# Splitting the second MoE layer's weights in another order, and waiting for the last scatters on another engine

## The reference

```
attn: scores = q k^T / 8;  keep scores >= max - tau;  softmax;  times v        4 x 8 heads, 576 x 64
moe : expert = argmax(xn @ en^T / tau);  out = gate * relu(x @ w1[e]) @ w2[e]   2304 tokens, 512 -> 1024 -> 512, 8 experts
last: h = x @ w_in;  g = h * tanh(log1p(exp(min(h, 20))));  out = g @ w_out      2304 tokens, 512 -> 2048 -> 512
```

## Time and profile before

| | |
|---|---|
| median of three runs | 1065.5 us |
| the profiled execution's own time | 1065.5 us |
| its span | 1063.9 us |
| PE busy | 1023.2 us (96%) |
| DVE / ACT / POOL busy | 625.7 / 505.5 / 587.7 us |
| mean granted TensorE clock | 0.987 of full |

### The profile page before, as it was taken

How to read it: one execution, slowest core, us unless ns; L and a number is a source line. 1 busy time by engine, 2 the same in 40 slices (tenths; PEclk the granted TensorE clock), 3 DMA queues, 4 the chain that set the end, 5 groups by cost and what they waited for, 6 DMA issues and landing times.

```text
span 1063.9 us, 20987 instructions
## 1 busy us (share of the span) xinstructions
PE 1023.2 (96%) x6712; PEld 850.1 (80%) x6712; DVE 625.7 (59%) x1484; ACT 505.5 (48%) x1020; POOL 587.7 (55%) x672
## 2 busy tenths in 40 slices
PE   7999999999966999899999999999999999999996
PEld 5777777777634888788888889999999999999995
DVE  6998989898764222122222226776676676666653
ACT  5777777777653222222222224555545545555442
POOL 3344444444345868677660627776556565565564
PEclk9999999999987999999999999999999999999999
DMA  8165425441065899998871736400000100000000
GB/s 200 40 169 161 120 81 152 127 125 44 12 220 149 247 287 279 293 295 266 291 240 47 264 104 208 119 31 21 27 14 31 31 10 20 30 30 0 9 22 31
DMA packets 97526, 128.87 MB, mean 121 GB/s; under 512 B 34400, under 2 KB 51808, under 8 KB 96928
## 3 DMA queue, kind: packets, MB, share of 16 engines
q1 hardware_dynamic: 72544, 66.54, 21.8%
q0 software_dynamic: 18880, 53.22, 15.8%
q10 hardware_dynamic: 6016, 7.96, 2.1%
HBM read 111.70 MB, written 16.00 MB: 120 GB/s over the span
## 4 chain that ended last, share of the span: by engine, by line
PE 59%; POOL 4%; DMA 4%; issue 2%; DVE 2%; ACT 1%; another core or an unknown queue 0%; POOLq 0%; SPq 0%; ACTq 0%; DVEq 0%
PE ps L1110 18%; PE ps L1111 18%; PE ps L1112 18%; DMA stage<-w 4%; POOL wl L594 3%; PE ps L1136 1%; PE ps L1048 1%; POOL wh L605 1%; PE ps L1185 1%; PE ps L1106 1%; POOL xs_far L631 1%; PE ps L1058 1%; ACT junk L824 1%; PE ps L997 0%
## 5 line engine op out<-in xcount | busy, mean ns | idle before, releaser
L594 POOL TENSOR_TENSOR wl<-stage,wh 128x512 fp32r<-128x512 f32 x128 | 162.8, 1294 | 56.0 <-DMA stage<-w 50.1
L708 POOL TENSOR_TENSOR mg<-mw,mr 128x384 f32<-128x384 f32 x96 | 117.3, 1222 | 73.7 <-DVE mr L1545 73.2
L766 ACT ACTIVATE ex<-sc,rmin 128x576 f32<-128x576 f32 x144 | 111.6, 776 | 78.0 <-DVE sc L1316 78.0
L714 POOL TENSOR_TENSOR gl<-mg,gh 128x384 fp32r<-128x384 f32 x96 | 98.6, 1028 | 79.1 <-ACT gh L902 78.2
L1110 PE MATMUL ps<-yth,winh 128*128 128x384 f32 x384 | 130.9, 341 | 0.0
L1112 PE MATMUL ps<-yth,winl 128*128 128x384 f32 x384 | 129.5, 337 | 0.0
L1111 PE MATMUL ps<-ytl,winh 128*128 128x384 f32 x384 | 128.8, 335 | 0.0
L1326 DVE SCALAR_TENSOR_TENSOR pm<-sc,thr,ex 128x576 f32<-128x576 f32 x144 | 116.7, 812 | 19.2 <-POOL thr L558 15.3
L1316 DVE TENSOR_SCALAR_CACHE_REDUCE sc<-ps,nscale 128x576 f32<-128x576 f32 x144 | 116.9, 813 | 9.8 <-PE ps L957 9.0
L558 POOL TENSOR_SCALAR thr<-rmin,taup 128x1 f32<-128x1 f32 x144 | 75.4, 524 | 76.2 <-DVE sc L1316 74.2
L1111 PE MATMUL ps<-woutl,gh 128*128 128x512 f32 x288 | 113.5, 394 | 0.0
(11 more groups left out here) (193 smaller groups left out, 2253.0 us busy)
## 6 DMA issues: line engine op xcount, KB each, us to landing
stage<-w SPq DMA_DIRECT2D x128, 256.0 KB, 4.5
wh<-w POOLq DMA_DIRECT2D x32, 1024.0 KB, 8.1
y_dense<-yo ACTq DMA_DIRECT2D x25, 256.5 KB
q_t<-qT SPq DMA_DIRECT2D x16, 288.0 KB, 3.6
k_t<-kT SPq DMA_DIRECT2D x16, 288.0 KB, 4.1
vb<-v SPq DMA_DIRECT2D x16, 288.0 KB, 4.5
stage<-w_in SPq DMA_DIRECT2D x16, 256.0 KB, 3.4
winh<-w_in POOLq DMA_DIRECT2D x1, 4096.0 KB, 13.8
```

Of the source, the lines that this page charges most:

```text
L594: g.tensor_tensor(dst, raw, src.bitcast(F32), ALU.subtract).then_inc(w_split, 1)
L708: g.tensor_tensor(mg[:, f % 2, :], mw[:, f % 2, :], mr[:, f % 2, :], ALU.mult).then_inc(g_done, 1)
L714: g.tensor_tensor(gl[:, f % 4, :], mg[:, f % 2, :], gh[:, f % 4, :].bitcast(F32), ALU.subtract).then_inc(gl_ready, 1)
L766: act.activation(ex[:, i % 2, t * S:(t + 1) * S], sc[:, i % 2, t * S:(t + 1) * S], ACT.Exp, bias=rmin[:, i % 2, t:t + 1], scale=-1.0).then ...
```

## The change

Five edits. On SP, the reload `load_y(1)` (the next group's tokens) is issued before chunk 4 of w_out and no longer before chunk 8. On POOL, four chunks and no longer eight are split before the first group; chunks 4 to 15 follow one in each of the iterations f = 0 to 11 (before: chunks 8 to 15 in f = 6 to 13). `load_w_out(2)` moves, with its wait for `m2_done`, from f = 4 to f = 2, ahead of chunk 6; `load_w_out(3)` moves to just ahead of chunk 8, also f = 4. On DVE, `result(24)` moves from ahead of `mish_n(3)` and `weigh(3)` to behind them. The waits for `out_stored` move from SP's end to POOL's end.

```diff
@@ sync
         for c in range(CH_E):
-            if c == 2 * CQ:
+            if c == CQ:
                 load_y(1)
             chunk(CH_E * (E + 1) + c, c, wout_c[c])
         for gi in range(2, NG):
             load_y(gi)
-        for j in range(GT_):
-            sp.wait_ge(out_stored[j], 16 * NG)
@@ gpsimd
         def w_out_low(c):
+            if c == CQ + 2:
+                g.wait_ge(m2_done, SLOTS)
+                load_w_out(2)
+            if c == 2 * CQ:
+                load_w_out(3)
             low_parts(CH_E // STAGES * (E + 1), ...
@@ group, gpsimd
-                if first and f == LAG:
-                    g.wait_ge(m2_done, SLOTS)
-                    load_w_out(2)
-                    load_w_out(3)
-                if first and LAG + 2 <= f < LAG + 2 + 2 * CQ:
-                    w_out_low(f + 2)
+                if first and f + CQ < NF:
+                    w_out_low(f + CQ)
@@
-        for c in range(2 * CQ):
+        for c in range(CQ):
             w_out_low(c)
@@ end of gpsimd
+        for j in range(GT_):
+            g.wait_ge(out_stored[j], 16 * NG)
@@ group, vector
+                mish_n(c, f)
+                weigh(c, f)
                 if first and f == HEAD - 1:
                     result(SLOTS - 1)
-                mish_n(c, f)
-                weigh(c, f)
```

## The result

The changed kernel is slower. Its median is 1076.85 us (ten runs, 1070.65 to 1078.91), that of the kernel before, on the same chip, 1066.89 us (ten runs, 1061.99 to 1070.43). The ratio on record, of the mean of all 35 runs of the changed kernel to the mean of these ten, is 1.0083, with a 95% interval of 1.0064 to 1.0102; the two medians alone would give 1.0093. That is 6.8 to 10.9 us more. The predicted range ended 5.4 us above the kernel before. The profiled execution took 1076.51 us, its span 1074.9.

What follows compares the result with a forecast made beforehand. It took PE, busy throughout, as the bound, so only new gaps and the end could count. Against 1065.5 us: +2.8 stall, +1.6 clock, -2.9 drain, +1.5 in sum, giving 1067.0 us; range 1062.8 to 1070.9.

Steps and rivals of the forecast that it cites:

- The bound: From 644 to 1055 us PE is busy throughout at full clock, so work brought forward gains nothing.
- The stall: PE ahead of down(0): it stands 2.8 us, because result(24) comes late.
- The chain: From m2_done on POOL through load_w_out(2), a split, gated(1), then DVE's weigh(3) and result(24), to PE's down(0) at 662.4.
- The lock-out of DVE and POOL: mish_n(3) and the split exclude each other; stall 3.0 us by that rule, 2.7 by the median; allowed 0.1 us.
- The clock: PE behind the stall: half clock for a while, +1.6 us, with a chance of 0.55.
- The drain: POOL's drain at the kernel's end, started with nothing in flight, lasts 0.17 us: the end comes 2.9 us earlier.
- the choice of the nearest row: For POOL's last drain, the length of the only other POOL drain, 171 ns at the start, was taken.
- Rival 3: POOL's last drain is work of its own, 4.8 us from its start: end +1.7 us, 1071.6 or 1070.0 us; chance 0.14.
- The splits in f = 0 to 11: POOL iterations 1.3 us longer, no cost: f = 6 to 13 showed none, and PE moved back by the stall.
- The cover of chunk 4: Chunk 4 lands at 652, so POOL's work ends at about 657.4, before it must be free at 657.86.
- rival 4: The passage ahead of down(0) doesn't stall and only the drain counts: 1062.6 us; chance 0.06.

Runs made afterwards that it cites:

- e_act_first: The changed kernel with ACT doing exp_u(3) ahead of high_g(1); by the runs +6.5 us (4.4 to 8.6) against the kernel before.
- e_end_only: The kernel before with only the waits for out_stored moved from SP's end to POOL's; by the runs +3.2 us (1.4 to 4.9) against the kernel before.
- v_drains_spread: The kernel before with two added POOL drains, six w_out splits up front and chunks 6 and 7 split in f = 3 and f = 5; ratio 0.9982.
- e_drain_before: The kernel before with one POOL drain added just ahead of its last three scatters; by the runs -0.4 us (-2.1 to 1.3).
- e_drain_idle: The kernel before with one POOL drain added ahead of copy_ids(0, 0), where POOL waits for data; by the runs -1.4 us (-3.6 to 0.8).
- v_drains: The kernel before with two POOL drains added, ahead of the last layer's first ids and of the last three scatters; ratio 0.9986.
- e_splits_late_y: The kernel before with the change's earlier splits, load_y(1) still ahead of chunk 8, m2_done wait and load_w_out(2) ahead of chunk 7; by the runs +2.3 us.
- e_end_back: The changed kernel with the waits for out_stored back on SP; ratio 1.0084 to the kernel before.
- e_load_later: The changed kernel with the m2_done wait and load_w_out(2) ahead of chunk 7, not 6; by the runs +5.3 us (3.1 to 7.5) against the kernel before.

## Why the prediction was wrong

The bound held: PE was the path, nothing brought forward could gain, and only new gaps, the clock behind them and the end could move the time. Three terms were off, one of them in sign, and the reason for a fourth, at nothing, does not hold.

1. **The stall, +2.8, was 4.98.** The chain was right from `m2_done` to `gated(1)`: the load comes 0.69 us after the last m2 matmul (predicted 0.48), the split and `gated` end 3.74 after it (predicted 3.57), and `weigh` with `result` takes 1.27 (1.28). Missing is what lies between them. The prediction took `mish_n(3)` as started at about 658.4; but it needs `exp_u(3)`, and on ACT that is queued behind `high_g(1)`, which waits for `gated(1)`. From `gated(1)` ending (663.09) to `weigh(3)` (665.25) this costs 2.16 us: `high_g(1)`, `exp_u(3)`, and a `mish_n(3)` of 1.12 us where 0.55 is its median. What is queued behind the wait was named on POOL and on DVE, but not on ACT, the third engine that it reaches. e_act_first, with that queue changed, took 1.7 us of it away. The lock-out of DVE and POOL, for which the prediction allowed 0.1 us, rests on the same wrong start of `mish_n(3)`; where `mish_n(3)` did start that early, in e_act_first, it lasted 2.99 us.
2. **The clock, +1.6, was 2.06 (b).** It fell, as forecast; the loss is larger because `down(0)` ran at half clock from its first matmul on, and lost 1.92 us by itself.
3. **The drain, -2.9, was +1.99.** The step that failed is the choice of the nearest row: the 171 ns drain at the program's start was the same instruction with another past, no DMA of POOL's ahead of it. Late in the kernel it is 4.73 us with nothing in flight, and e_end_only isolates its price, +2.01. Rival 3 had +1.7, from 4.8 us behind a landing 1.72 us past the last issue (1058.88 to 1060.6); the other 0.3 us is that the drain starts 2.03 us past it (1067.89 to 1069.92), behind the landing and POOL's three waits.
4. **The splits in f = 0 to 11, at nothing.** In the changed kernel they showed no gap. That PE had moved back by 5 us and covered them, as the prediction argued, fits this. But its other reason, that splits in f = 6 to 13 had cost nothing, does not carry: without the stall they cost 2.05 us.

The cover of chunk 4 held: it was there at 652.07 (predicted 652), and POOL was idle for 2.46 us ahead of `m2_done`. With 4.98 + 2.06 + 1.99 the sum is +9.03 instead of +1.5. Rival 3 with the clock's fall, at 1071.6 us, had the signs of all three terms right; its chance was 0.08, and it lay outside the range. The range's lower end, 1062.8, was called rival 4, whose own sum is 1062.6; nothing hangs on that.

Left open: what decides whether `mish_n` is held, by which route the dense splits cost 2.05 us, and why the stall near 444 us varies.

## What to carry to other kernels

When a wait is moved ahead of work, follow that work's readers on every engine until the chain closes, the engine that only converts or looks up included: in an in-order stream, one late reader holds whatever is queued behind it. An iteration that just fits (4.20 against 4.17 us) has no room to absorb one more issue; extra work is safer with the loads in an iteration left free, as in v_drains_spread. And before the waits at a kernel's end are moved, look at which engine's drain is the longest. POOL's, here, took its time from when POOL came to it, so it belongs as early as possible, and most of it could be paid in advance in an idle stretch.

## What was not expected of the hardware

**POOL's drain grows with what POOL has done since its last drain**, even with nothing in flight. The third column is the time since that drain's end (or since the first one, at 0.7 us). The last is the time from the end of POOL's last instruction (in the changed kernel, from the drain's start behind the last landing) to the drain's end. It is read from the trace's own times, since the views show a start to 0.1 us only:

| drain | POOL's DMAs since the last one | us since the last one | us |
|---|---|---|---|
| before, last | 80 | 1058 | 4.74 |
| changed, last (nothing in flight) | 80 | 1069 | 4.73 |
| e_drain_before, added | 77 | 1050 | 4.51 |
| e_drain_idle, added | 58 | 610 | 4.10 |
| e_drain_idle, last | 22 | 440 | 2.71 |
| v_drains, second added | 19 | 433 | 1.64 |
| e_drain_before, last (ends at about the landing) | 3 | 4 | 1.91 |
| v_drains, last (ends at about the landing) | 3 | 5 | 1.91 |

That an earlier drain shortens the last one is shown. That the count of DMAs sets the length is not: the time since the last drain falls with it in this table, and so does POOL's other work; no run separates them. Nor does either fall on one line: 19 and 22 DMAs differ by 1.1 us at nearly the same time, and the expectation for the former was 2.6. Those two differ also in that three scatters were just issued ahead of the latter.

The Trainium skill (VectorE: DVE Perf Modes, "The DRAIN you can't avoid") gives the drains around a kernel as constant at about 12 ns on all engines. In this case's traces SP's 13 ns in the kernel before agrees; SP's 128 ns in the changed kernel does not, and none of POOL's does.

**DVE can be held through several POOL instructions.** `mish_n` reads one tile of SBUF as both of its inputs, and its median in the last layer is 0.55 us. Four times it lasted 2.99 to 3.40 us: at 668.99 in the changed kernel, at 659.64 and 667.79 in e_act_first, at 662.28 in e_splits_late_y. Each time it had begun 0.09 to 0.48 us after the start of a DMA issue of POOL, with a split and `gated` following without a pause, and each time it ended 0.42 or 0.43 us behind the end of `gated`.

The Trainium skill (SBUF — State Buffer, on the shared port pair) says that such an instruction and one of GpSimd that reads SBUF exclude each other for the whole instruction. The trace agrees that DVE is held, but through two such instructions in a row, split and `gated`, and not for one. It is a matter of a few hundredths of a microsecond: in e_end_back, with the same code in this passage as the changed kernel, `mish_n` began at 667.93, 0.08 us into the issue, and took 0.56 us. What decides it is not shown.

**The clock behind a gap of 2 us went either way.** In the last layer it fell to half at or behind gaps of 4.82, 3.13 and 2.00 us, and stayed full behind 2.07 and 1.57 us. Gaps in the experts stage of the same traces fit in: it fell behind 2.32 us (442.09 in v_drains) and 3.10 us (341.51 in e_end_back), and stayed full behind 1.70 us (e_load_later) and 1.62 us (the changed kernel). The gaps of 2.00 and 2.07 us were each seen once.
